# First tiles of a fused convolution and feed-forward kernel: one DMA for each load, w_in in four pieces, second convolution by GpSimd alone

## The chip, the cores and the metric

The kernel runs on one core of one Trainium2 chip. The metric is the device time of one execution in microseconds (us). Before the change it was 1414.38 us, the median of three runs (1413.4 to 1414.79 us).

## What is computed

Everything is float32. Sixteen thousand tokens (4 sequences of 4096) of width 192 go through a causal convolution whose seven taps differ for each token and each of eight heads, and then through a feed-forward layer with a rational activation:

```python
w = softmax(weight_gen)                      # over the 7 taps, per token and head
x_pad = concatenate([zeros(B, 6, D), x])     # each sequence starts with six zero tokens
out = einsum('bshk,bskhg->bshg', w, x_unf)   # x_unf: the seven tokens up to this one
h = out @ w_in                               # 192 -> 2048
P = a[0] + a[1]*h + a[2]*h**2 + a[3]*h**3
Q = 1 + |b[0]|*|h| + |b[1]|*h**2
return (P / (Q + 1e-6)) @ w_out              # 2048 -> 192
```

## The kernel before

**Layout.** Partition p of the 128 holds 128 consecutive tokens; a tile is four of them on every partition (512 tokens), and there are 32 tiles. To convolve a tile the kernel needs its four tokens and the six before them, a window of ten tokens (`xwin`, two buffers). From the third tile on, a window is one DMA of ten consecutive tokens of each partition's row (`load_x`, L273). For the first tile the six tokens before it belong to the neighbouring partition's row, or are zeros where a sequence starts. So the first tile is loaded by one DMA of four tokens (L262) and four DMAs of six tokens, each over 31 partitions (`load_halo`, L245); the second tile by one DMA of eight tokens (L267) and four of two tokens over 31 partitions. DVE writes the zeros first (L511, L512).

**First product.** x and w_in are each split into a high and a low fp32r part, and h is the sum of five products of such parts (L680). Row `wi_stage[:, 0]` holds the first 128 input rows of w_in and `wi_stage[:, 1]` the last 64 twice. It is loaded in two halves of the 2048 units, three DMAs each (`load_wi`, L254). For each half ACT copies the high part (`wi_hi`, L438), and DVE subtracts it to get the low part (`wi_lo`, L563).

**Groups.** The 16 chunks of 128 units go in six groups q of 3, 2, 3, 3, 2 and 3 chunks. For each group PE makes h in PSUM, ACT makes |h| (L474, or L479), a square (L477) and a linear term (L482), DVE finishes the numerator (L623, L626, whose end, `h_used`, frees the PSUM banks), and the denominator is summed by a DMA that GpSimd issues (groups 0, 2, 3, 5: `den` plus `beta`, L350) or by GpSimd and DVE (groups 1, 4: L357, L631). ACT inverts it two groups later (Ln L455, Exp L458), DVE forms the gate three groups later (L607), and PE multiplies it with w_out four groups later (`back`, L690).

**Convolution.** Each tile's convolution has 13 steps, seven products (L327) and six additions (L331). GpSimd does them for tile t + 2 in between its work for the groups of tile t. Only the first two tiles are convolved ahead of the loop, and there the 32 heads of a partition's four tokens are split: DVE takes 22 of the first tile (528 columns) and 12 of the second (288 columns) in `pre_conv` (L545, L556), GpSimd the rest (240 and 480 columns). The convolved tile is transposed by PE in two parts: `transpose1` (L665) and `transpose0` (L658). ACT then copies their high parts (`hi_part1` L424, `hi_part0` L419) and DVE makes the low parts (L575, L569).

**What sets the order ahead of the loop.** Each engine runs its instructions in program order, with semaphores between them.

- SP: taps 0 and 1, tokens of tile 0, its four halo DMAs, taps 2 (after `pre_sub` 1, the first taps' subtraction), first half of w_in, tokens and halos of tile 1, second half, w_out, taps 3, and the window of tile 2 once the first convolution is over. The window of tile 3 waits for the second convolution.
- DVE: softmax start (L519 maximum, L522 subtraction) for tiles 0 and 1, softmax end (L529, L532, L534) for both, `pre_conv(0)`, three tiny instructions for `root` (L585 to L590), `wi_lo` of the first half, softmax start of tile 2, the low parts of tile 0, `wi_lo` of the second half, softmax end of tile 2, `pre_conv(1)`, and then tile 0's groups.
- ACT: exponentials of taps 0 and 1 (L414), small values, both halves of `wi_hi`, high parts of tile 0, the exponential of taps 2 (which waits for `pre_sub` 3, L441), and then tile 0's groups.
- GpSimd: its part of convolutions 0 and 1, and then tile 0's groups with convolution 2.
- PE: the transposes of tile 0 after both parts of convolution 0, then the groups. In the first tile, the group with number `FIRST_XT1` = 2 begins with `transpose1` of tile 1, after both parts of convolution 1, and `hi_part1` on ACT and `lo_part1` on DVE stand one group earlier (L484, L616).

Every group q of 2 or more in tile 0 waits on PE for `h_used` of the group two before it (L705).

Of the kernel before, what the change touches and what calls it, by code (L numbers as in the profile page):

```python
# [18 lines left out]


# [6 lines left out]
ALU = mybir.AluOpType  # L27
# [18 lines left out]
FIRST_XT1 = 2  # L46


def conv_rational_ffn(nc, x, weight_gen, w_in, w_out, a, b, out):
    B, S, D = x.shape  # L50
    HEADS, TAPS = weight_gen.shape[2:]
    HEAD_DIM = D // HEADS
    FF = w_in.shape[1]
# [12 lines left out]
    SEQ_PARTS = S // PER_PART  # L66
    assert sum(GROUP_CHUNKS) == CHUNKS and D1 == 64 and COLS == 512

    x_rows = x.rearrange("b s d -> (b s d)")
    x_part = x_rows.rearrange("(p e) -> p e", p=P)  # L70
# [3 lines left out]
    def before(tokens):  # L74

        start = (PER_PART - tokens) * D
        return x_rows[start:start + (P - 1) * PER_PART * D].rearrange("(p e) -> p e", p=P - 1)[:, 0:tokens * D]

    ctx = ExitStack()
    with ctx:  # L80
# [72 lines left out]
        wi_loaded = [sem(f"wi_loaded{n}") for n in range(2)]  # L153
# [5 lines left out]
        halo_zero = sem("halo_zero")  # L159
# [47 lines left out]
        def after_dmas(s, parity, more=0):  # L207


            return 8 * s + (16 - 8 * parity + 16 * more)  # L210
# [20 lines left out]
        DVE_HEADS = (22 * NH // 32, 12 * NH // 32)  # L231
        SEQS = P // SEQ_PARTS
        HALO_DMAS = SEQS

# [4 lines left out]
        def _(sp):  # L239
            def load_halo(n, tokens):  # L240

                sp.wait_ge(halo_zero, n + 1)
                for q in range(SEQS):
                    rows = slice(q * SEQ_PARTS + 1, (q + 1) * SEQ_PARTS)
                    sp.dma_start(xwin[n][rows, 0:tokens * D],  # L245
                                 before(tokens)[rows.start - 1:rows.stop - 1, :]).then_inc(x_loaded[n], 16)

            def load_wi(half):

                units = slice(half * FF // 2, (half + 1) * FF // 2)  # L250
                for to, frm in ((wi_stage[:, 0, units], w_in[0:P, units]),
                                (wi_stage[0:D1, 1, units], w_in[P:D, units]),
                                (wi_stage[D1:P, 1, units], w_in[P:D, units])):
                    sp.dma_start(to, frm).then_inc(wi_loaded[half], 16)  # L254
# [4 lines left out]
            ahead = HALO - TOK  # L259
            sp.dma_start(taps_raw[0][:, :], taps_part[:, 0:TAPW]).then_inc(taps_loaded[0], 16)  # L260
            sp.dma_start(taps_raw[1][:, :], taps_part[:, TAPW:2 * TAPW]).then_inc(taps_loaded[1], 16)
            sp.dma_start(xwin[0][:, HALO * D:], x_part[:, 0:ROW]).then_inc(x_loaded[0], 16)  # L262
            load_halo(0, HALO)
            sp.wait_ge(pre_sub, 1)
            load_taps(2, 0)
            load_wi(0)
            sp.dma_start(xwin[1][:, ahead * D:], x_part[:, 0:2 * ROW]).then_inc(x_loaded[1], 16)  # L267
            load_halo(1, ahead)
            load_wi(1)
            sp.dma_start(wo[:, :, :], w_out.rearrange("(c p) d -> p c d", p=P)).then_inc(wo_loaded, 16)  # L270

            def load_x(s, parity):
                sp.dma_start(xwin[parity][:, :],  # L273
                             x_part[:, bass.ds(s * ROW - HALO * D, (TOK + HALO) * D)]).then_inc(x_loaded[parity], 16)

            sp.wait_ge(pre_sub, 2)
            load_taps(3, 1)
            sp.wait_ge(conv_steps, CONV_STEPS)
# [7 lines left out]
            def tile(t, odd, first=False, more_x=True, more_taps=True):  # L286
# [6 lines left out]
                if more_x:  # L293
                    sp.wait_ge(conv_steps, CONV_STEPS * (t + 2))
                    if first:
                        sp.wait_ge(conv_by_dve, 2 * CONV_STEPS)
                    load_x(t + 3, 1 - odd)
# [15 lines left out]
        def _(pool):  # L313
# [58 lines left out]
            def tile(t, odd, first=False, conv_ahead=True, taps_ahead=True):  # L372
                done = CONV_STEPS * (t + 2)
                start = 1 if first else 0
                for q in range(GROUPS):
# [8 lines left out]
                    if conv_ahead:  # L384
                        if q == start:
# [4 lines left out]
                            pool.wait_ge(x_loaded[odd], after_dmas(t + 2, odd, HALO_DMAS))  # L390
# [17 lines left out]
        def _(act):  # L408
# [26 lines left out]
            for half in range(2):  # L435
                units = slice(half * FF // 2, (half + 1) * FF // 2)
                act.wait_ge(wi_loaded[half], 3 * 16)
                act.activation(wi_hi[:, :, units], wi_stage[:, :, units], ACT.Copy).then_inc(wi_hi_ready, 1)  # L438
# [21 lines left out]
            def tile(t, odd, first=False, second=False, xt_ahead=True, taps_ahead=True):  # L460
                for q in range(GROUPS):
# [18 lines left out]
                    if first and q == 0:  # L480
                        act.wait_ge(wi_lo_ready, 2)
# [27 lines left out]
        def _(dve):  # L509

            dve.memset(xwin[0][:, 0:HALO * D], 0.0).then_inc(halo_zero, 1)  # L511
            dve.memset(xwin[1][:, 0:(HALO - TOK) * D], 0.0).then_inc(halo_zero, 1)  # L512
# [24 lines left out]
            def pre_conv(s):  # L537

                count = DVE_HEADS[s]
                cols = slice(0, count * HEAD_DIM)  # L540
                done = s * CONV_STEPS

                def product(k):
                    to = heads(dprod[k % 3]) if k else heads(conv[s])
                    dve.tensor_tensor(to[:, 0:count, :], shifted(xwin[s], k)[:, 0:count, :],  # L545
                                      tap(taps[s], k)[:, 0:count, :], ALU.mult).then_inc(conv_by_dve, 1)
# [218 lines left out]
```

## Time and profile before

| | before |
|---|---|
| median of the runs | 1414.38 us |
| the profiled execution, its own time | 1414.09 us |
| its span, first to last instruction | 1412.3 us |
| PE / ACT / DVE / GpSimd busy, share of the span | 93% / 89% / 85% / 74% |
| granted TensorE clock, mean | 0.993 of full |
| bytes moved by DMA | 152.21 MB |

The profile is of one execution; its times are counted from the span's start. Busy shares are averages over the whole span, and say nothing about how the first 100 us differ from the rest. "L245" is line 245 of the kernel. PE stands for TensorE's matmuls and transposes, PEld for its weight loads, POOL for GpSimd, SPq for the issuing of DMAs by SyncE.

### The profile page before, as it was taken

The numbers are of one execution on the slowest core, as the hardware profiler recorded it, in microseconds if no ns is written. First come the engines' busy times: TensorE is split into PE (matmuls) and PEld (weight loads), VectorE is DVE, ScalarE is ACT, GpSimd is POOL, SyncE is SP. The second block draws the span as 40 slices with busy tenths as digits, with TensorE's granted clock in tenths as the row PEclk, the third lists the DMA queues.
The fourth block names the chain that finished last, engine by engine and source line by source line (L and its number), as shares of the span: only waits on it lengthen the run. The fifth ranks groups of instructions, "written<-read, shape, count | busy, mean of one in ns | idle before, by whom it ended". The sixth has DMA issues, their size and how long they took to land.

```text
span 1412.3 us, 19121 instructions
## 1 busy us (share of the span) xinstructions
PE 1307.0 (93%) x6912; PEld 1174.9 (83%) x6912; DVE 1201.9 (85%) x841; ACT 1253.8 (89%) x1030; POOL 1040.7 (74%) x672
## 2 busy tenths in 40 slices
PE   0279999999999999999999999999999999999997
PEld 0268898888889888889888888988888898888887
DVE  2989888888988889988888998888889888899775
ACT  0379999999999999999999999999999999999995
POOL 1879787778878778877877887877788787787210
PEclk9889999999999999999999999999999999999999
DMA  2445544544545554454454455445445445533432
GB/s 89 134 93 119 115 112 109 131 93 98 131 101 117 117 126 87 109 129 97 109 131 113 88 121 114 112 109 131 93 97 131 103 115 117 123 84 78 100 68 67
DMA packets 35486, 152.21 MB, mean 108 GB/s; under 512 B 3992, under 2 KB 10260, under 8 KB 35472
## 3 DMA queue, kind: packets, MB, share of 16 engines
q0 software_dynamic: 18432, 100.67, 36.1%
q1 hardware_dynamic: 16752, 51.36, 10.9%
q8 instruction: 7, 0.11, 0.0%
q14 instruction: 7, 0.06, 0.0%
q10 hardware_dynamic: 288, 0.00, 0.0%
HBM read 38.78 MB, written 12.58 MB: 36 GB/s over the span
## 4 chain that ended last, share of the span: by engine, by line
PE 62%; ACT 26%; issue 7%; SPq 2%; DVE 2%; POOL 1%; DMA 1%; ACTq 0%; DVEq 0%; POOLq 0%
PE ops L690 32%; PE hps L680 28%; ACT num L482 7%; ACT beta L477 6%; ACT den L455 5%; ACT den L474 4%; ACT out_sb L449 2%; SPq L245 1%; PE hps L665 1%; DMA num<-in_moe_w_in 1%; SPq L254 1%; ACT den L458 1%; DVE gate L545 0%; POOL conv L331 0%; POOL prod L327 0%
## 5 line engine op out<-in xcount | busy, mean ns | idle before, releaser
L690 PE MATMUL ops<-wo,gate 128*128 128x192 f32 x4096 | 700.7, 327 | 33.0 <-ACT out_sb L449 29.4
L690 PEld LDWEIGHTS ops<-wo,gate 128*128 128x128 f32 x4096 | 674.4, 190 | 60.3 <-issue 42.0
L623 DVE TENSOR_TENSOR num<-num,hps 128x1536 f32<-128x1536 f32 (+1 forms) x192 | 301.5, 1570 | 157.6 <-ACT num L482 157.6
L331 POOL TENSOR_TENSOR conv<-conv,prod 128x768 f32<-128x768 f32 (+2 forms) x192 | 396.2, 2064 | 15.0
L607 DVE SCALAR_TENSOR_TENSOR gate<-num,coef,den 128x1536 f32<-128x1536 f32 (+1 forms) x192 | 402.8, 2098 | 2.4 <-issue 1.4
L327 POOL TENSOR_TENSOR prod<-xwin,taps 128x768 f32<-128x768 f32 (+2 forms) x192 | 334.1, 1740 | 3.5
L626 DVE SCALAR_TENSOR_TENSOR num<-num,coef,hps 128x1536 f32<-128x1536 f32 (+1 forms) x192 | 314.2, 1637 | 6.8
L350 POOL DMA_DIRECT2D den<-beta x128 | 112.9, 882 | 256.6 <-ACT beta L477 248.7
L482 ACT ACTIVATE num<-hps,coef 128x1536 f32<-128x1536 f32 (+1 forms) x192 | 288.6, 1503 | 0.0
L474 ACT ACTIVATE den<-hps,absb 128x1536 f32<-128x1536 f32 x128 | 197.1, 1540 | 87.1 <-PE hps L680 87.1
L458 ACT ACTIVATE den<-den 128x1536 f32<-128x1536 f32 (+1 forms) x192 | 259.4, 1351 | 4.2
L455 ACT ACTIVATE den<-den 128x1536 f32<-128x1536 f32 (+1 forms) x192 | 261.0, 1360 | 0.0
L680 PE MATMUL hps<-xt_hi,wi_hi 128*128 128x512 f32 x512 | 226.3, 442 | 3.9 <-ACT xt_hi L419 3.9
L680 PE MATMUL hps<-xt_hi,wi_lo 128*128 128x512 f32 x512 | 203.8, 398 | 0.0
L680 PE MATMUL hps<-xt_hl,wi_hi 128*128 128x512 f32 x512 | 203.3, 397 | 0.0
L680 PE MATMUL hps<-xt_lo,wi_hi 128*128 128x512 f32 x512 | 202.7, 396 | 0.0
L680 PE MATMUL hps<-xt_hl,wi_lo 128*128 128x512 f32 x512 | 202.2, 395 | 0.0
L477 ACT ACTIVATE beta<-hps,root 128x1536 f32<-128x1536 f32 x128 | 197.1, 1540 | 0.0
L357 POOL TENSOR_SCALAR beta<-den,absb 128x1024 f32<-128x1024 f32 x64 | 139.4, 2179 | 38.2 <-ACT den L479 22.2
L680 PEld LDWEIGHTS hps<-xt_hl,wi_hi 128*128 128x128 f32 x512 | 96.8, 189 | 24.1
L680 PEld LDWEIGHTS hps<-xt_lo,wi_hi 128*128 128x128 f32 x512 | 96.6, 189 | 24.2 <-DVE xt_lo L569 0.4
L680 PEld LDWEIGHTS hps<-xt_hl,wi_lo 128*128 128x128 f32 x512 | 96.7, 189 | 22.9
(50 smaller groups left out, 728.9 us busy)
## 6 DMA issues: line engine op xcount, KB each, us to landing
den<-beta POOLq DMA_DIRECT2D x128, 768.0 KB, 5.8
xwin<-in_x SPq DMA_DIRECT2D x30, 960.0 KB
out<-out_sb SPq DMA_DIRECT2D x32, 384.0 KB, 4.2
taps_raw<-in_weight_gen SPq DMA_DIRECT2D x32, 112.0 KB, 3.9
wo<-in_moe_w_out SPq DMA_DIRECT2D x1, 1536.0 KB, 14.9
num<-in_moe_w_in SPq DMA_DIRECT2D x2, 512.0 KB, 6.8
num<-in_moe_w_in SPq DMA_DIRECT2D x4, 256.0 KB, 8.7
xwin<-in_x SPq DMA_DIRECT2D x1, 768.0 KB
```

Source lines behind the costliest of these rows:

```text
L327: pool.tensor_tensor(to[:, first_head:, :], shifted(xwin[parity], k)[:, first_head:, :], tap(taps[parity], k)[:, first_head:, :], ALU.mult ...
L331: pool.tensor_tensor(conv[parity][:, cols], conv[parity][:, cols], prod[k % 2][:, cols], ALU.add).then_inc(conv_steps, 1)
L455: act.activation(slot(den, g), slot(den, g), ACT.Ln, bias=1.0 + 1e-6).then_inc(ln_ready, 1)
L458: act.activation(slot(den, g), slot(den, g), ACT.Exp, scale=-1.0).then_inc(inv_q_ready, 1)
L474: act.activation(slot(den, g), h_of(q), ACT.Abs, scale=absb[:, 0:1]).then_inc(abs_ready, 1)
L477: act.activation(slot(beta, g), h_of(q), ACT.Square, scale=root[:, 2:3]).then_inc(square_ready, 1)
L482: act.activation(slot(num, g), h_of(q), ACT.Identity, scale=coef[:, 3:4], bias=coef[:, 2:3]).then_inc(lin_ready, 1)
L607: dve.scalar_tensor_tensor(slot(gate, g), slot(num, g), coef[:, 0:1], slot(den, g), ALU.add, ALU.mult).then_inc(gate_ready, 1)
L623: dve.tensor_tensor(slot(num, g), slot(num, g), h_of(q), ALU.mult).then_inc(num2_ready, 1)
L626: dve.scalar_tensor_tensor(slot(num, g), slot(num, g), coef[:, 1:2], h_of(q), ALU.add, ALU.mult).then_inc(h_used, 1)
L680: last = pe.matmul(to, w, xt[:, :], start=(m == 0), stop=(m == len(terms) - 1))
L690: last = pe.matmul(ops[:, j // 2, (j % 2) * D:(j % 2 + 1) * D], gate[:, g % GATE_RING, n * COLS + j * P:n * COLS + (j + 1) * P], wo[:, c, ...
```

## The change

The host code in `kernel()` now builds two arrays before the launch: `x_windows`, in which each partition's row is its 128 tokens with the six before them (zeros at the start of a sequence) ahead of them, and `stacked(w_in)`, in which the last 64 rows stand twice, beside the first 128. All loads of x are then one DMA of ten tokens from each row, and w_in is loaded in four pieces of 512 units, one DMA each. The zeros, the halo DMAs and their waits go. The order of SP's loads, the split of the first two convolutions, DVE's order and `FIRST_XT1` change as shown.

```diff
-FIRST_XT1 = 2
+FIRST_XT1 = 3
...
+    PIECES = 4
+    PIECE = FF // PIECES
...
-        DVE_HEADS = (22 * NH // 32, 12 * NH // 32)
+        DVE_HEADS = 22 * NH // 32
...
+            def load_wi(piece):
+                units = slice(piece * PIECE, (piece + 1) * PIECE)
+                sp.dma_start(wi_stage[:, :, units], w_in[:, :, units]).then_inc(wi_loaded[piece], 16)
+
+            def load_x(s, parity):
+                sp.dma_start(xwin[parity][:, :],
+                             x_windows[:, bass.ds(s * ROW, (TOK + HALO) * D)]).then_inc(x_loaded[parity], 16)
...
+            load_taps(0, 0)
+            load_x(0, 0)
+            load_taps(1, 1)
+            load_wi(0)
+            load_wi(1)
+            load_x(1, 1)
+            load_wi(2)
+            load_wi(3)
             sp.wait_ge(pre_sub, 1)
             load_taps(2, 0)
...
             sp.wait_ge(pre_sub, 2)
             load_taps(3, 1)
+            sp.dma_start(wo[:, :, :], w_out.rearrange("(c p) d -> p c d", p=P)).then_inc(wo_loaded, 16)
             sp.wait_ge(conv_steps, CONV_STEPS)
             sp.wait_ge(conv_by_dve, CONV_STEPS)
             load_x(2, 0)
...
             for s in range(2):
                 pool.wait_ge(pre_taps, s + 1)
-                pool.wait_ge(halo_zero, 2)
-                pool.wait_ge(x_loaded[s], after_dmas(s, s, HALO_DMAS))
+                pool.wait_ge(x_loaded[s], after_dmas(s, s))
                 for n in range(CONV_STEPS):
-                    conv_step(s, n, s, s * CONV_STEPS, DVE_HEADS[s])
+                    conv_step(s, n, s, s * CONV_STEPS, DVE_HEADS if s == 0 else 0)
...
+            for piece in range(PIECES):
+                units = slice(piece * PIECE, (piece + 1) * PIECE)
+                act.wait_ge(wi_loaded[piece], 16)
                 act.activation(wi_hi[:, :, units], wi_stage[:, :, units], ACT.Copy).then_inc(wi_hi_ready, 1)
...
                     if first and q == 0:
-                        act.wait_ge(wi_lo_ready, 2)
+                        act.wait_ge(wi_lo_ready, PIECES)
...
-            dve.memset(xwin[0][:, 0:HALO * D], 0.0).then_inc(halo_zero, 1)
-            dve.memset(xwin[1][:, 0:(HALO - TOK) * D], 0.0).then_inc(halo_zero, 1)
...
             pre_softmax_end(0, 0)
             pre_softmax_end(1, 1)
-            pre_conv(0)
+            pre_conv()
+            wi_lo_piece(0)
+            lo_part1(0, 0, hps[:, BANK1, :])
+            lo_part0(0, 0)
             dve.wait_ge(root_guess, 1)
...
-            wi_lo_half(0)
+            for piece in range(1, PIECES):
+                wi_lo_piece(piece)
             dve.wait_ge(conv_steps, CONV_STEPS)
             pre_softmax_start(2, 0)
-            lo_part1(0, 0, hps[:, BANK1, :])
-            lo_part0(0, 0)
-            wi_lo_half(1)
             pre_softmax_end(2, 0)
-            pre_conv(1)
...
                 for n in range(GROUP_CHUNKS[q]):
+                    if first:
+                        pe.wait_ge(wi_lo_ready, (GROUP_START[q] + n) * P // PIECE + 1)
...
+def windows_of(x):
+    B, S, D = x.shape
+    per_part = B * S // P
+    padded = np.zeros((B, S + HALO_TOKENS, D), x.dtype)
+    padded[:, HALO_TOKENS:] = x
+    rows = [padded[n, s:s + per_part + HALO_TOKENS] for n in range(B) for s in range(0, S, per_part)]
+    return np.stack(rows).reshape(P, (per_part + HALO_TOKENS) * D)
+
+def stacked(w_in):
+    return np.stack([w_in[0:P], np.concatenate([w_in[P:], w_in[P:]])], axis=1)
```

PE's and SP's waits for DVE's part of the second convolution go too. `pre_conv()` is `pre_conv(0)` under another name.

## Rows read from the trace of the kernel before

**Rows 1.** The chain that ended last, stretches 0 to 110 and 100 to 200: start, us, what.

```profile
37.31 11.21 DMA num<-in_moe_w_in
...
69.25 1.76 DVE num L623
...
109.11 0.60 PE hps L665 x4
...
150.88 0.44 PE hps L665 x4
```

**Rows 2.** Busy time by stretch, first row: the columns' names.

```profile
core 0: us, PE busy (x) PEld busy (x) DVE busy (x) ACT busy (x) POOL busy (x), PEclk, DMA share, GB/s
...
24.00:26.00 2.00, 0.00 (x0) 0.00 (x0) 0.00 (x0) 0.00 (x0) 0.00 (x0) 1.00 0.06 25
...
120.00:162.90 42.90, 42.15 (x226) 37.79 (x225) 38.57 (x27) 40.34 (x34) 35.26 (x23) 1.00 0.48 109
```

**Rows 3.** Instructions in order of time, the start: start, us, engine, operation [idle before].

```profile
5.60 0.39 DVE L519 TENSOR_REDUCE tap_max<-taps_raw 128x32 f32<-128x224 f32 x1 [1.28 <-DMA taps_raw<-in_weight_gen]
...
8.30 0.39 DVE L534 TENSOR_TENSOR taps<-taps,tap_inv 128x224 f32<-128x224 f32 x1
```

**Rows 4.** DMA rate in 40 slices of the stretch 108 to 124.

```profile
GB/s 0 0 0 0 0 269 38 173 461 422 422 442 353 230 215 200 230 215 215 169 230 138 41 0 0 0 0 0 0 0 0 20 0 0 0 0 0 0 0 0
```

**Rows 5.** Instructions in order of time, first convolution and what follows it.

```profile
31.61 0.71 DVE L545 TENSOR_TENSOR conv<-xwin,taps 128x528 f32<-128x528 f32 x1 [22.92 <-DMA xwin<-in_x]
...
42.88 2.22 DVE L556 TENSOR_TENSOR conv<-conv,gate 128x528 f32<-128x528 f32 x2
...
44.61 1.03 POOL L331 TENSOR_TENSOR conv<-conv,prod 128x240 f32<-128x240 f32 x1
...
45.76 2.28 DVE L563 TENSOR_TENSOR wi_lo<-num,wi_hi 128x2048 fp32r<-128x2048 f32 x1
...
50.16 1.20 POOL L331 TENSOR_TENSOR conv<-conv,prod 128x480 f32<-128x480 f32 x1
...
50.97 0.69 DVE L575 TENSOR_TENSOR xt_hl<-hps,xt_hl 64x512 fp32r<-64x512 f32 x1 [1.79 <-ACT xt_hl L424]
...
52.30 2.31 DVE L563 TENSOR_TENSOR wi_lo<-num,wi_hi 128x2048 fp32r<-128x2048 f32 x1
...
52.54 3.14 POOL L331 TENSOR_TENSOR conv<-conv,prod 128x480 f32<-128x480 f32 x1
...
57.15 1.54 ACT L474 ACTIVATE den<-hps,absb 128x1536 f32<-128x1536 f32 x1 [5.46 <-PE hps L680]
```

**Rows 6.** Instructions in order of time, 65 to 100.

```profile
65.91 1.00 POOL L350 DMA_DIRECT2D den<-beta  x1
...
73.30 0.57 POOL L382 TENSOR_TENSOR taps<-taps_raw,tap_max 128x224 f32<-128x224 f32 x1 [5.14 <-DVE tap_max L634]
73.84 1.54 POOL L327 TENSOR_TENSOR conv<-xwin,taps 128x768 f32<-128x768 f32 x1
...
77.08 1.85 POOL L331 TENSOR_TENSOR conv<-conv,prod 128x768 f32<-128x768 f32 x1
...
78.51 1.55 ACT L474 ACTIVATE den<-hps,absb 128x1536 f32<-128x1536 f32 x1 [3.85 <-PE hps L680]
...
82.09 0.89 POOL L350 DMA_DIRECT2D den<-beta  x1 [3.16 <-ACT beta L477]
...
82.89 1.49 ACT L455 ACTIVATE den<-den 128x1536 f32<-128x1536 f32 x1
...
85.92 1.54 ACT L474 ACTIVATE den<-hps,absb 128x1536 f32<-128x1536 f32 x1
...
89.48 0.88 POOL L350 DMA_DIRECT2D den<-beta  x1 [3.02 <-ACT beta L477]
```

**Rows 7.** GpSimd's DMA at 110.97, from issue to landing.

```profile
DMA to landing us min/median/max: 8.0/8.0/8.0
```

More of the change, by code:

```diff
@@ L21 @@
+import numpy as np
 import concourse.bass as bass
@@ L45, with conv_rational_ffn @@
 XT0, XT1 = 4, 1
-FIRST_XT1 = 2
-def conv_rational_ffn(nc, x, weight_gen, w_in, w_out, a, b, out):
-    B, S, D = x.shape
+FIRST_XT1 = 3
+def conv_rational_ffn(nc, x_windows, weight_gen, w_in, w_out, a, b, out):
+    B, S = weight_gen.shape[:2]
+    D = w_out.shape[1]
     HEADS, TAPS = weight_gen.shape[2:]
     HEAD_DIM = D // HEADS
-    FF = w_in.shape[1]
+    FF = w_in.shape[2]
     PER_PART = B * S // P
@@ L152, in conv_rational_ffn @@
         small_loaded = sem("small_loaded")
-        wi_loaded = [sem(f"wi_loaded{n}") for n in range(2)]
+        wi_loaded = [sem(f"wi_loaded{n}") for n in range(PIECES)]
         wo_loaded = sem("wo_loaded")
@@ L205, in conv_rational_ffn, with after_dmas @@
         pe_passed = sem("pe_passed")
-        def after_dmas(s, parity, more=0):
-            return 8 * s + (16 - 8 * parity + 16 * more)
+        def after_dmas(s, parity):
+            return 8 * s + (16 - 8 * parity)
         def wait_q(engine, t, q):
@@ L239, in _ @@
         def _(sp):
[L240 to L254, printed above, removed]
+            def load_wi(piece):
+                units = slice(piece * PIECE, (piece + 1) * PIECE)
+                sp.dma_start(wi_stage[:, :, units], w_in[:, :, units]).then_inc(wi_loaded[piece], 16)
@@ L268, in _ @@
[L268 to L274, printed above, removed]
             sp.wait_ge(pre_sub, 2)
             load_taps(3, 1)
+            sp.dma_start(wo[:, :, :], w_out.rearrange("(c p) d -> p c d", p=P)).then_inc(wo_loaded, 16)
@@ L554, in pre_conv, with wi_lo_piece @@
                         product(k + 1)
-                    dve.wait_ge(conv_by_dve, done + 2 * k)
-                    dve.tensor_tensor(conv[s][:, cols], conv[s][:, cols], dprod[k % 3][:, cols],
+                    dve.wait_ge(conv_by_dve, 2 * k)
+                    dve.tensor_tensor(conv[0][:, cols], conv[0][:, cols], dprod[k % 3][:, cols],
                                       ALU.add).then_inc(conv_by_dve, 1)
-            def wi_lo_half(half):
-                units = slice(half * FF // 2, (half + 1) * FF // 2)
-                dve.wait_ge(wi_hi_ready, half + 1)
+            def wi_lo_piece(piece):
+                units = slice(piece * PIECE, (piece + 1) * PIECE)
+                dve.wait_ge(wi_hi_ready, piece + 1)
                 dve.tensor_tensor(wi_lo[:, :, units], wi_stage[:, :, units], wi_hi[:, :, units].bitcast(F32),
@@ L677, in first_product @@
                     for m, (w, xt) in enumerate(terms):
-                        if very_first and n == 0 and m == 2:
+                        if first and q == 0 and n == 0 and m == 2:
                             pe.wait_ge(xt_lo_ready, 2)
@@ L705, in tile @@
                         pe.wait_ge(h_used, i - 1)
-                    if first and GROUP_START[q] == CHUNKS // 2:
-                        pe.wait_ge(wi_lo_ready, 2)
                     if xt_ahead and q == (FIRST_XT1 if first else XT1):
                         pe.wait_ge(conv_steps, CONV_STEPS * (t + 2))
-                        if first:
-                            pe.wait_ge(conv_by_dve, 2 * CONV_STEPS)
                         pe.sem_inc(pe_passed, 1)
@@ L717, in tile @@
                         transpose0(1 - odd)
-                    first_product(q, odd, first and q == 0)
+                    first_product(q, odd, first)
                     if first and q == LAG:
@@ L754 @@
     nc = bacc.Bacc("TRN2", target_bir_lowering=False, num_devices=1)
+    B, S, D = inputs["x"].shape
+    laid_out = {"x_windows": windows_of(inputs["x"]), "weight_gen": inputs["weight_gen"],
+                "w_in": stacked(inputs["moe_w_in"]), "w_out": inputs["moe_w_out"],
+                "a": inputs["moe_a"], "b": inputs["moe_b"]}
     arrays, args = {}, []
-    for name in _INS:
-        v = np.ascontiguousarray(inputs[name])
+    for name, value in laid_out.items():
+        v = np.ascontiguousarray(value)
         arrays[f"in_{name}"] = v
         args.append(nc.dram_tensor(f"in_{name}", v.shape, mybir.dt.from_np(v.dtype), kind="ExternalInput").ap())
-    B, S, D = inputs["x"].shape
     out = nc.dram_tensor("out_0", (B * S, D), F32, kind="ExternalOutput").ap()
```

46 lines of the change are left out of this document (10 added, 36 removed).

## The prediction, made before the changed kernel was run

> **What bounds the kernel now.** Two parts have to be told apart. In the body, PE is the bound: between 120 and 163 us it is busy for 42.15 of 42.90 us at full clock [rows 2], and the chain of waits goes through the transposes of a new tile at 109.11 and again at 150.88 [rows 1], so a tile costs 41.8 us there. The diff leaves a tile's instructions in the body alone: the loads of x keep their size, and only their source rows move. So I look at the part ahead of it, and read the chain, then the stretches, then the instructions in order of time.
>
> The start is bound by loads. Both engines start the first convolution at about 31.6 us, and DVE had been idle for 22.92 us, until x came [rows 5]. Between 24 and 26 us no engine works, and the DMA engines move 25 GB/s at a share of 0.06, one sixteenth [rows 2]: the halo DMAs of 31 partitions run on one of 16 engines. Behind them SP can't issue, so w_in is late too: its last DMA lands 11.21 us after 37.31, at 48.5 us, and the chain passes through it [rows 1]. After that comes DVE's share of the second convolution, which holds its first work on group 0 of tile 0 until 69.25 us [rows 1], though ACT had begun that group at 57.15 [rows 5]. ACT gets group 2 at 78.51 [rows 6], and from there the same sequence runs into the body. So every us by which ACT reaches group 3 (85.92 [rows 6]) earlier should come off the span, as long as GpSimd keeps up.
>
> **The change, part by part.** All times below are from the span's start.
>
> Loads. Taps 0, x of tile 0 (960 KB) and taps 1 are issued first, each on 128 partitions. Before, taps 1 had landed at 5.60 with a 384 KB load of x beside it [rows 3]. Now 0.59 MB more lies ahead of it; a window of this size, just after SP issued it, moved at 422 GB/s and more [rows 4], which makes 1.4 us, and it is issued one place later, some 0.4 us. I take 7.3 us; bounds are 5.6 us (as before) and 9.6 us (the extra bytes at half that rate, and everything late by another 1.1 us). The Trainium skill (DMA: Bandwidth & Descriptors, Anatomy of one DMA) fits a GpSimd DMA as 2.0 us plus bytes at 436 GB/s; as an estimate, the 1.2 MB up to taps 1 would be there at 5.5 us, and the sum would gain 1.8 us more. The first rows of this trace speak against taking it, since 112 KB took until 5.60.
>
> The rest of the loads (w_in in 2 MB, the second window, some 3 MB in all) needs 7 us at 422 GB/s and 15 at half of that. All of it is there by 23 us at the latest, before anything below asks for it; its cover is the first convolution. w_out comes later still, but is asked for only at group 4. The two zeroings on DVE (1.4 us) were hidden behind the taps, so taking them away is worth nothing.
>
> First convolution. From taps 1 at 5.60 to the end of the second softmax at 8.69 are 3.1 us [rows 3]: DVE starts at 10.4 instead of 31.61. GpSimd needs only the first softmax and starts some 1.1 us sooner. The two engines hold each other up: a DVE step takes 0.71 us with GpSimd idle and 1.1 beside it, and a GpSimd addition of 480 columns took 3.14 us instead of 1.20 when it met the 2.31 us of `wi_lo` [rows 5]. So they take turns. DVE's 13 steps took from 31.61 to 45.10, 13.5 us [rows 5]. GpSimd, two steps ahead, finishes at 10.4 + 14.0 - 2.0 = 22.4 and goes on to full width, so DVE's last two steps wait for steps of 1.6 us instead of 0.5: 1.0 us more. DVE ends at 24.9.
>
> DVE's queue after it. It is now on the path, since ACT's first work on tile 0 stands behind the exponential of taps 2, which waits for DVE's subtraction of taps 2, which stands behind all four pieces of `wi_lo`. A piece takes half of 2.28 us [rows 5], 1.15, and each waits for a full-width step of GpSimd (product 1.62 from start to start, addition 1.93 [rows 6]). Piece 0: 1.25 + 1.15, to 27.3. Low parts of tile 0: 1.33, from 50.97 to 52.30 [rows 5], to 28.6; PE and ACT have made the transposes and high parts meanwhile. `root`: 0.66, from 45.10 to 45.76 [rows 5], to 29.3. Pieces 1 to 3: three turns of 1.15 + 1.7, less some of the first wait, 8.2, to 37.5. Maximum, wait and subtraction: 1.9, to 39.4. Exponential 0.4: ACT starts group 0 at 39.9 instead of 57.15.
>
> Tile 0. Group 0 takes ACT 4.4 us (78.51 to 82.89 for three such operations [rows 6]), so DVE starts its numerator at 44.3; its convolution no longer stands in the way (before: 69.25). From there to ACT's group 2 were 9.26 us, with 0.60 for the transposes of tile 1 [rows 1, 6], which now come a group later: 8.7, so 53.0 against 78.51. From group 2 to group 3 were 7.41 us (78.51 to 85.92 [rows 6]); now ACT's high part of tile 1 (0.6) stands between: group 3 starts at 61.0 against 85.92. **That is 24.9 us earlier.**
>
> GpSimd. Its second convolution is 7 products and 6 additions of full width: 7 x 1.62 + 6 x 1.93 = 22.9 us. Four pieces of `wi_lo` add 0.9 each (1.94 us were added by one of twice the size [rows 5]) and DVE's last two steps 0.35 each: 27.3, from 22.4 to 49.7. Its DMA for group 0 stands behind that. Such DMAs land after 5.8 us usually, but after 8.0 when a window of x was issued just before [rows 7], and here SP issues tile 3's window at the same moment: 57.7. ACT wants it after group 2, at 53.0 + 4.4 + 0.6 = 58.0. So it is just in time, and this is what is late next. After it, GpSimd starts the third convolution at 52.5 (of the 7.4 us from its DMA at 65.91 to 73.30, 5.14 were a wait [rows 6]), which is 3.6 us late against 73.84 - 24.9; its next waits for ACT, 3.16 and 3.02 us [rows 6], take that up.
>
> Sum: 1414.09 (the profiled execution's own time) - 24.9 = 1389.2 us. That execution lay 0.3 us under the median, so no correction.
>
> **The rivals.**
>
> *No holding up.* If DVE doesn't wait for GpSimd's full-width steps, DVE's queue loses 1.0 + 1.25 + 4.7 + 1.5 = 8.4 us. GpSimd then ends at 22.4 + 22.9 = 45.3, its DMA lands at 53.3 and becomes the bound: 4.7 us more gained, 1384.5; with a landing after 6.5 us, 1383.0. The rows of the first convolution and of 3.14 us speak against it; for it speaks only that the turns might fall better than I drew them.
>
> *GpSimd decides.* If each of the 13 steps is held as the ones beside `wi_lo` are, the convolution takes 22.9 + 13 x 0.9 = 34.6 us and ends at 57.0, the DMA lands at 65.0, and ACT waits 7 us for it: 1396.2. DVE has little to do between 40 and 44 us, which speaks against so much.
>
> *The new load goes to one DMA engine,* as the halos do: then 983 KB at 25 GB/s [rows 2] take 39 us, x of tile 0 is there at 42.5 instead of 31.6, everything shifts by 32 us against my sum, and the kernel ends at 1421.3, slower. It decides from a landing of about 35 us on. Against it: the same shape in the body moved at 422 GB/s [rows 4]. The Trainium skill (DMA: Bandwidth & Descriptors, Why a DMA increments its semaphore by 16 and not by 1) says that a DMA goes to the largest number of engines up to 16 which divides its outer dimension, 1 for 31 rows and 16 for 128; the share of 0.06 agrees, and by it this rival doesn't happen.
>
> *The start is hidden anyway.* If the body had idle time to absorb it, nothing would change: 1414. PE at 98% leaves no room [rows 2].
>
> **How the numbers follow.** Forecast 0.55, no holding up 0.20, GpSimd decides 0.20, one engine 0.03, hidden 0.02. The range runs from 1383.5 to 1396.5 and holds the bounds of the landing (-1.7 and +2.3 us) within the first three cases. A measurement here tells 0.2% (2.8 us) from no change; the first three cases are all beyond that: faster 0.95, same 0.02, slower 0.03.
>
> **What would show it.** In the profile after: DVE's first convolution step near 10 us; no stretch of 25 GB/s; `wi_lo` steps longer than 1.15 us, with GpSimd steps between; ACT's first `den` of tile 0 near 40 us, its idle time before the exponential of taps 2 ended by DVE's subtraction; the last step of GpSimd's second convolution near 50 us; ACT's `den` of group 3 near 61; tile periods unchanged at 41.8 us. It is wrong if the first `den` comes near 31 (no holding up), if ACT's first Ln waits long for GpSimd's DMA (GpSimd decides), or if a later tile loses what the start gained.

## The result, and the profile after

The changed kernel takes 1391.74 us (median of four runs, 1391.33 to 1392.87), against 1414.17 us for the kernel before: a ratio of 0.9843, 95% interval 0.9826 to 0.986. That is 22.4 us less; 24.9 were forecast, and 1391.74 lies in the range of 1383.5 to 1396.5. The profiled execution had a span of 1391.0 us and took 1392.87 us itself, the slowest of the four; the last section says why. Two executions further below, one of kernel E and one of the kernel before beside it, took over 1900 us at a granted clock of 0.66 and are left out of the medians.

The first rows to read are the changed kernel's first 24 us (busy time by stretch; the columns are those of [rows 2]).

```profile
2.00:4.00 2.00, 0.00 (x0) 0.00 (x0) 0.00 (x0) 0.03 (x1) 0.00 (x0) 1.00 0.73 106
4.00:6.00 2.00, 0.00 (x0) 0.00 (x0) 0.78 (x2) 0.39 (x1) 0.00 (x0) 1.00 0.85 327
6.00:8.00 2.00, 0.00 (x0) 0.00 (x0) 0.00 (x0) 0.00 (x0) 0.00 (x0) 1.00 0.96 314
...
10.00:12.00 2.00, 0.00 (x0) 0.00 (x0) 1.90 (x6) 0.86 (x3) 1.32 (x2) 1.00 1.02 397
...
20.00:22.00 2.00, 0.00 (x0) 0.00 (x0) 2.00 (x3) 0.00 (x0) 1.84 (x3) 1.00 0.56 181
22.00:24.00 2.00, 0.00 (x0) 0.00 (x0) 2.00 (x3) 0.00 (x0) 1.92 (x3) 1.00 0.02 7
```

The stretches of 25 GB/s at a share of 0.06 are gone: the DMA engines are nearly full until almost everything has come, at about 22 us. SP isn't held up behind the halos any more either. In the kernel before, the issue of one load of taps behind them had taken 5.38 us, where the first loads took 0.4 us each:

```profile
8.55 5.38 SPq L257 DMA_DIRECT2D taps_raw<-in_weight_gen  x1
```

The instructions in order of time show what the engines made of it.

```profile
8.56 0.39 DVE L494 TENSOR_REDUCE tap_max<-taps_raw 128x32 f32<-128x224 f32 x1 [3.74 <-DMA taps_raw<-in_weight_gen]
...
11.57 1.11 DVE L518 TENSOR_TENSOR conv<-xwin,taps 128x528 f32<-128x528 f32 x1
...
23.34 3.15 DVE L529 TENSOR_TENSOR conv<-conv,gate 128x528 f32<-128x528 f32 x2
23.93 2.00 POOL L305 TENSOR_TENSOR conv<-xwin,taps 128x768 f32<-128x768 f32 x1
...
26.42 2.56 DVE L536 TENSOR_TENSOR wi_lo<-num,wi_hi 128x1024 fp32r<-128x1024 f32 x1
...
30.85 7.77 DVE L536 TENSOR_TENSOR wi_lo<-num,wi_hi 128x1024 fp32r<-128x1024 f32 x3
...
40.85 1.52 ACT L451 ACTIVATE den<-hps,absb 128x1536 f32<-128x1536 f32 x1
...
45.43 1.75 DVE L595 TENSOR_TENSOR num<-num,hps 128x1536 f32<-128x1536 f32 x1 [3.15 <-ACT num L459]
...
49.16 1.83 POOL L309 TENSOR_TENSOR conv<-conv,prod 128x768 f32<-128x768 f32 x1
...
50.92 1.01 POOL L327 DMA_DIRECT2D den<-beta  x1
```

DVE's first step of the convolution stood at 31.61 before [rows 5] and is at 11.57 now. The last two steps of its share take 3.15 us for the two, where they took 2.22 beside GpSimd's short steps. A piece of `wi_lo` takes 2.56 us and three take 7.77, for 1.15 us of work each: DVE and GpSimd lengthen each other, as if they took turns. The chain that ended last says what decides after that (start, us, what).

```profile
49.92 1.01 issue
50.92 9.70 DMA den<-beta
60.62 0.02 issue
60.64 1.48 ACT den L432
...
63.78 1.43 ACT den L451
...
71.80 1.19 POOL beta L334
72.99 2.49 POOL prod L305
...
84.90 1.82 POOL conv L309
86.73 0.14 issue
86.86 0.60 PE hps L637 x4
```

It runs through GpSimd's second convolution, then 9.70 us of the DMA of group 0, then ACT, and from 71.80 through GpSimd again to the transposes of tile 2 at 86.86, which came at 109.11 before [rows 1]: 22.25 us earlier. From there on both kernels do the same in the same time, 41.5 us from one copy of an output tile to the next, up to the last tile. That one takes 32.3 us in this trace and 31.0 in that of before, so that about 1 us of the gain is missing again at the end of this execution.

### The profile page after: what moved, and what is told of

It is laid out like the page before. It is cut to its first block, busy times and chain, and to the rows that moved or that the text cites. A ratio compares the mean times of both kernels' runs of the same rounds, so it can differ in the third digit from the quotient of the medians.

```text
span 1391.0 us, 19098 instructions
## 1 busy us (share of the span) xinstructions
PE 1310.3 (94%) x6912; PEld 1177.7 (85%) x6912; DVE 1194.8 (86%) x828; ACT 1253.9 (90%) x1032; POOL 1046.6 (75%) x672
## 4 chain that ended last, share of the span: by engine, by line
PE 62%; ACT 26%; issue 7%; POOL 4%; DMA 1%; DVE 0%; SPq 0%; ACTq 0%; POOLq 0%; DVEq 0%
PE ops L664 33%; PE hps L654 28%; ACT num L459 7%; ACT beta L454 6%; ACT den L432 6%; ACT den L451 4%; POOL conv L309 2%; ACT out_sb L426 2%; POOL prod L305 2%; PE hps L637 1%; DMA den<-beta 1%; ACT den L435 1%; DMA taps_raw<-in_weight_gen 0%; ACT taps L391 0%; POOL conv L305 0%
## 5 line engine op out<-in xcount | busy, mean ns | idle before, releaser
L664 PE MATMUL ops<-wo,gate 128*128 128x192 f32 x4096 | 702.1, 328 | 32.8 <-ACT out_sb L426 29.3
L595 DVE TENSOR_TENSOR num<-num,hps 128x1536 f32<-128x1536 f32 (+1 forms) x192 | 301.5, 1570 | 158.8 <-ACT num L459 158.7
L309 POOL TENSOR_TENSOR conv<-conv,prod 128x768 f32<-128x768 f32 (+1 forms) x192 | 399.7, 2082 | 15.0
L579 DVE SCALAR_TENSOR_TENSOR gate<-num,coef,den 128x1536 f32<-128x1536 f32 (+1 forms) x192 | 402.4, 2096 | 2.7 <-issue 1.3
L305 POOL TENSOR_TENSOR prod<-xwin,taps 128x768 f32<-128x768 f32 (+1 forms) x192 | 338.7, 1764 | 3.4
L654 PEld LDWEIGHTS hps<-xt_hi,wi_hi 128*128 128x128 f32 x512 | 97.5, 190 | 27.1 <-DVE num L598 11.4
```

What stands on the lines that cost most here:

```text
L305: pool.tensor_tensor(to[:, first_head:, :], shifted(xwin[parity], k)[:, first_head:, :], tap(taps[parity], k)[:, first_head:, :], ALU.mult ...
L309: pool.tensor_tensor(conv[parity][:, cols], conv[parity][:, cols], prod[k % 2][:, cols], ALU.add).then_inc(conv_steps, 1)
L579: dve.scalar_tensor_tensor(slot(gate, g), slot(num, g), coef[:, 0:1], slot(den, g), ALU.add, ALU.mult).then_inc(gate_ready, 1)
L595: dve.tensor_tensor(slot(num, g), slot(num, g), h_of(q), ALU.mult).then_inc(num2_ready, 1)
L654: last = pe.matmul(to, w, xt[:, :], start=(m == 0), stop=(m == len(terms) - 1))
L664: last = pe.matmul(ops[:, j // 2, (j % 2) * D:(j % 2 + 1) * D], gate[:, g % GATE_RING, n * COLS + j * P:n * COLS + (j + 1) * P], wo[:, c, ...
```

## Experiments

Ten more kernels were run, each beside the kernel before, and the changed kernel and K a second time (mostly five executions each; eleven of P, four of EF). The medians are blurred by the last tile, so the traces are read at two marks: the transposes of tile 2 ("T2"), and ACT's first copy of an output tile ("copy"), which closes the start. A group's `den` is the start of ACT's first instruction on it. All times in us:

| kernel | median | first conv. step | group 0's den | group 2's den | group 0's DMA: issue, landing after | group 3's den | T2 | copy |
|---|---|---|---|---|---|---|---|---|
| before | 1414.17 | 31.61 | 57.15 | 78.51 | 65.91, 6.5 | 85.92 | 109.11 | 132.28 |
| changed | 1391.74 | 11.57 | 40.85 | 54.22 | 50.92, 9.7 | 63.69 | 86.86 | 110.04 |
| changed, again | 1392.08 | 11.70 | 40.97 | 55.80 | 51.05, 10.0 | 64.09 | 87.45 | 110.60 |
| A loads alone | 1391.74 | 9.47 | 36.22 | 57.39 | 43.17, 6.1 | 64.80 | 88.10 | 111.25 |
| P GpSimd alone | 1414.45 | 31.87 | 58.19 | 79.42 | 72.71, 9.9 | 86.82 | 110.03 | 133.21 |
| B split back | 1392.95 | 11.58 | 38.10 | 57.98 | 43.76, 5.9 | 65.86 | 90.50 | 113.67 |
| C taps 1 first | 1390.35 | 9.41 | 37.77 | 52.23 | 49.63, 9.7 | 62.43 | 85.57 | 108.72 |
| D tile 3's x later | 1389.42 | 11.61 | 40.88 | 55.67 | 50.96, 5.9 | 63.55 | 87.26 | 110.39 |
| E softmax early | 1392.77 | 11.41 | 35.47 | 52.13 | 50.66, 9.8 | 63.49 | 86.63 | 109.79 |
| F DMA early | 1391.94 | 11.51 | 40.78 | 55.39 | 44.38, 5.9 | 63.27 | 86.90 | 110.08 |
| EF both | 1393.45 | 11.51 | 35.97 | 51.10 | 43.74, 5.9 | 58.98 | 86.85 | 111.43 |
| I beta on ACT | 1392.02 | 11.49 | 40.75 | 55.44 | 50.83, 10.0 | 63.86 | 87.04 | 110.20 |
| K all four | 1391.93 | 9.72 | 33.29 | 50.84 | 40.70, 5.9 | 58.72 | 82.19 | 105.35 |
| K again | 1390.60 | 9.43 | 32.75 | 48.12 | 40.75, 5.9 | 57.30 | 84.54 | 110.38 |

Two yardsticks for small differences. The kernel before had a median of 1413.67 us beside A to D, 1414.72 beside P, E, F and EF, 1414.00 beside I and K, and 1414.51 beside the two repeats, so medians of different rounds differ by up to 1 us for no reason of the kernel. And the two traces of the changed kernel differ by 0.6 us at T2 and at the copy, and by 1.6 us at group 2's `den`; what is smaller than that in one trace is not a finding.

**A. The loads alone,** in the kernel before.

```diff
-            load_halo(0, HALO)
+            load_taps(0, 0)
+            load_taps(1, 1)
+            load_x(0, 0)
             sp.wait_ge(pre_sub, 1)
             load_taps(2, 0)
             load_wi(0)
...
+            load_x(1, 1)
             load_wi(1)
```

`x_windows` and `stacked(w_in)` are built as in the changed kernel, but w_in comes in two halves, one DMA each.

> The kernel before with its loads changed alone: windows and stacked w_in, one DMA each, in the old order (taps 0, taps 1, x of tile 0, taps 2, w_in in two halves around x of tile 1). The split of the second convolution, DVE's order and FIRST_XT1 = 2 stay. My theory (two chains: DVE's queue ahead of tile 0, and GpSimd's second convolution with its DMA for group 0): taps 1 lands at 5.6 us, the first convolution starts at 8.8 us instead of 31.6, the 1.8 us that ACT waited for the second half of w_in go too, and the rest of the old sequence follows unchanged, so DVE's first numerator starts at 44.5 instead of 69.25 and the kernel takes about 1389.7 us, 2 us less than with the whole change: the rest of the change costs what it gains or more. Rival (the parts are needed together, since DVE's 13 steps of the second convolution stand on the path): DVE's numerator not before 50 us, 1396 us or more.

Its median is 1391.74 us (ratio 0.984, 0.9827 to 0.9853), the very figure of the whole change. The rival falls: the numerator starts at 46.90, not after 50. The forecast was 2 us too low: taps 1 was there only at 6.4 us and x of tile 0 at 9.3, and DVE's steps of 288 columns took 1.3 to 1.5 us beside GpSimd's, where they took 0.45 alone. So the new loads carry all but about 1 us of the gain: A's T2 and copy come 0.7 to 1.2 us after those of the changed kernel's two traces. That the median is the same to the digit is chance. The rest of the diff isn't idle, though. A loads taps 1 ahead of x of tile 0, the changed kernel behind it; C below, the changed kernel with A's order of these two, has T2 and the copy 2.5 us before A. No run separates the windows of x from the stacked w_in, nor w_in's four pieces and `FIRST_XT1` = 3 from the rest.

**P. The second convolution by GpSimd alone,** in the kernel before.

```diff
-        DVE_HEADS = (22 * NH // 32, 12 * NH // 32)
+        DVE_HEADS = (22 * NH // 32, 0)
...
-            pre_conv(1)
```

PE's and SP's waits for DVE's part of it go too.

> The kernel before with one part of the change alone: the second convolution by GpSimd alone, DVE's 13 steps of it gone; loads, orders and FIRST_XT1 = 2 as before. My theory: DVE could start tile 0's numerator at 61.7 us instead of 69.25, but GpSimd's convolution, 46.4 us + 22.9 us of full-width steps + 3.4 us behind the two wi_lo, ends near 72.7 us, and the transposes of tile 1 wait for it there as they waited for the numerator before (72.97): no change, 1414 us within 1 us. Rival (DVE's queue was the bound): up to 7 us less, 1407 us.

As expected: 1414.45 against 1414.72 us, ratio 0.9998 (0.9989 to 1.0007). DVE's numerator starts at 62.79, but GpSimd ends at 72.7, and its DMA behind it, and PE's transposes, wait for that:

```profile
70.96 1.80 POOL L331 TENSOR_TENSOR conv<-conv,prod 128x768 f32<-128x768 f32 x1
72.71 1.00 POOL L350 DMA_DIRECT2D den<-beta  x1
72.83 0.61 PEld L664 LDWEIGHTS ops<-ident,conv 128*64 128x64 f32 x4 [12.79 <-issue]
```

**B. The second convolution split again,** in the changed kernel.

```diff
-                    conv_step(s, n, s, s * CONV_STEPS, DVE_HEADS if s == 0 else 0)
+                    conv_step(s, n, s, s * CONV_STEPS, DVE_HEADS[s])
...
             pre_softmax_end(2, 0)
+            pre_conv(1)
```

> The changed kernel with the second convolution split again, DVE taking 12 of 32 heads (288 columns) right after the second softmax part of tile 2, before tile 0's groups. My theory: DVE's first numerator starts some 3.5 us later (49 instead of 45.43), since DVE then works alone at about 0.45 us a step; GpSimd's part ends near 44 instead of 51, its DMA for group 0 lands in time, and ACT's wait of 1.5 us for it goes: 1393.7 us, 2 us more than the changed kernel. Rival (GpSimd's convolution alone sets the start): 1390 us or less.

1392.95 us. The steps came as expected (numerator at 48.95, DMA issued at 43.76 and landed after 5.9, no wait for it), and in its trace the copy is 3.6 us later than in the changed kernel; the median is 1.2 us above it, in the expected direction but smaller. GpSimd's convolution alone doesn't set the start. So the second convolution by GpSimd alone, worth nothing in the kernel before (P), is worth 3.1 to 3.6 us at the copy here, where DVE's 13 steps would stand ahead of its work on tile 0 and GpSimd's longer convolution is nearly hidden.

**C. Taps 1 before x.** Two lines of SP's list change places.

```diff
-            load_x(0, 0)
             load_taps(1, 1)
+            load_x(0, 0)
```

> The changed kernel with taps 1 issued before x of tile 0. My theory: taps 1 lands at 5.6 us instead of 8.5, x of tile 0 at about 8.6; both engines start the first convolution near 8.7 us; DVE starts 2.8 us earlier, GpSimd 1.9 us earlier and without its lead of one step, so DVE's last steps no longer meet full-width steps. The chain through GpSimd is 1.7 to 2.5 us shorter: 1389.7 us. Rival (x of tile 0 lands only at 10 us or later, and the taps were not what the start waited for): 1391.5 us.

Taps 1 is there at 6.1 instead of 8.6, x of tile 0 at 9.4, and the whole start moves by 1.3 us (T2 at 85.57, copy at 108.72); the median is 1390.35. Expected were 1.7 to 2.5; x comes later than I took it to, and now the convolution waits for it.

**D. Tile 3's window later.**

```diff
                     sp.wait_ge(conv_steps, CONV_STEPS * (t + 2))
+                    if first:
+                        sp.wait_ge(q_by_dma[0], 16)
                     load_x(t + 3, 1 - odd)
```

> The changed kernel, but SP issues the window of tile 3 only after the DMA of group 0 has landed, so that the two don't collide. My theory: that DMA lands after 6 us instead of 9.7, ACT's first Ln no longer waits for it (1.5 us), and then DVE's queue is the bound: 1.5 us less, 1390.2 us. Rival (GpSimd's chain alone decides, ACT follows it at once): 3.7 us less, 1388.0 us. Second rival (the collision is with something else, as w_out's or the taps' loads): DMA still over 8 us, no change.

The collision is what made the landing late: 5.9 us instead of 9.7, with the window and the taps behind it both issued after it, and ACT's first Ln doesn't wait any more. But group 2's `den`, which the landing can't touch, came 1.45 us later than in the changed kernel's first trace, so T2 and the copy are no earlier. Busy time by stretch shows why. The changed kernel:

```profile
50.00:52.00 2.00, 2.00 (x6) 1.52 (x6) 1.74 (x2) 0.00 (x0) 2.00 (x3) 0.50 0.15 15
52.00:54.00 2.00, 2.00 (x10) 1.55 (x9) 0.78 (x1) 0.00 (x0) 2.00 (x3) 0.99 0.86 184
```

and D:

```profile
50.00:52.00 2.00, 2.00 (x6) 1.52 (x6) 1.77 (x2) 0.00 (x0) 2.00 (x3) 0.50 0.00 0
52.00:54.00 2.00, 2.00 (x7) 1.52 (x6) 0.76 (x1) 0.00 (x0) 2.00 (x3) 0.50 0.85 169
```

In the second stretch the granted clock is 0.99 in one and 0.50 in the other, and 10 matmuls fall into it or 7. PE had been idle for 11 us before, and its 15 matmuls of group 2 begin at 1.2 GHz in both; when 2.4 GHz comes back differs from run to run. It isn't D's doing: in the changed kernel's own second trace the 15 matmuls took 6.5 us, as in D, where they had taken 5.1 in the first, and ACT waited only 0.28 us for the DMA instead of 1.46. Against that trace D reaches group 3 0.5 us earlier and T2 and the copy 0.2. The median, 1389.42, is 2.3 us below the changed kernel's; three of D's five executions (1388.8 to 1389.4) lie below all nine of the changed kernel (lowest 1390.8), the other two at 1392.6 and 1392.9, and the trace is of the last. The trace settles the collision, and the run times don't settle the gain.

**E, F and EF. Each chain shortened alone, and both.** E moves DVE's softmax start of tile 2 ahead of `wi_lo` pieces 1 to 3. F lets GpSimd issue the DMA of group 0 (`group(0, 0, 0, True)`) inside its second convolution, whose loop stands behind the definition of `group` there. EF is both. E's lines stand first below, F's behind them.

```diff
+            dve.wait_ge(conv_steps, CONV_STEPS)
+            pre_softmax_start(2, 0)
             for piece in range(1, PIECES):
                 wi_lo_piece(piece)
-            dve.wait_ge(conv_steps, CONV_STEPS)
-            pre_softmax_start(2, 0)
...
                     conv_step(s, n, s, s * CONV_STEPS, DVE_HEADS if s == 0 else 0)
+                    if s == 1 and n == 8:
+                        group(0, 0, 0, True)
...
-                    group(t, odd, q, first)
+                    if not first or q > 0:
+                        group(t, odd, q, first)
```

> The changed kernel with DVE's softmax start of tile 2 ahead of wi_lo pieces 1 to 3 instead of behind them. ACT's first den of tile 0 then comes at about 36 us instead of 40.85, but its linear term still waits for the fourth piece, so DVE's first numerator starts some 2 us earlier, at 43. My theory: ACT's first Ln waits for GpSimd's DMA of group 0, which lands at 60.6 as before, so nothing is gained: 1391.7 us within 0.5. Rival (DVE's queue ahead of tile 0 is the bound): 2.2 us less, 1389.5 us.

> The changed kernel with GpSimd issuing the DMA of group 0 after the ninth of the 13 steps of its second convolution instead of after all. My theory: it is issued near 44 us, lands near 50, ACT's first Ln doesn't wait (1.5 us less), the convolution ends 0.7 us later at no cost, and DVE's queue is then the bound: 1390.2 us, as with the window of tile 3 issued later. Rival (GpSimd's chain alone decides): 3 us or more less.

> The changed kernel with both: softmax start of tile 2 ahead of wi_lo pieces 1 to 3, and the DMA of group 0 after the ninth step. My theory of two chains nearly level: the first alone gives nothing, the second alone 1.5 us, both together 1.5 + 2.2 = 3.7 us, 1388.0 us. Rival (a third limit, GpSimd's later work or the TensorE clock, follows at once): together no more than the second alone, 1390.2 us.

E: ACT starts group 0 at 35.47 and then waits 3.36 us for the DMA, where it had waited 1.46; T2 stays (86.63), and the median is no lower (1392.77). The queue of DVE alone is not the bound. F: no wait for the DMA, but group 2 came 1.2 us later (its 15 products took 6.3 us instead of 5.1, at half clock for longer, as in D), so 0.4 us at group 3, nothing at T2 (86.90), and 1391.94; I had expected 1.5 less. The changed kernel's second trace has group 2 later still, so here too the clock hides what the edit is worth. EF: together they bring group 3 to 58.98, 4.7 us earlier, and still T2 stands at 86.85, and the median is 1393.45. My theory of two chains falls, and its rival, a third limit, holds. The waits and the instructions of EF name it:

```profile
65.19 0.86 POOL L320 DMA_DIRECT2D den<-beta  x1
65.80 1.83 POOL L305 TENSOR_TENSOR prod<-xwin,taps 128x768 f32<-128x768 f32 x1
67.70 2.90 POOL L309 TENSOR_TENSOR conv<-conv,prod 128x768 f32<-128x768 f32 x1
...
76.14 2.94 POOL L305 TENSOR_TENSOR prod<-xwin,taps 128x768 f32<-128x768 f32 x1
...
81.86 2.95 POOL L305 TENSOR_TENSOR prod<-xwin,taps 128x768 f32<-128x768 f32 x1
```

GpSimd has no wait left: it used to stand 3.3 us before the DMA of group 3 (67.22 in the changed kernel) and now comes there at 65.19 without standing. From that DMA to T2 it needs 19.6 us in the kernel before, the changed one, C and E, and 21.7 in EF, since its steps met more of DVE's instructions (2.9 us for steps that take 1.5 to 1.9 alone). That ACT's and DVE's lead is what put them there is argued, not shown: K's first trace, with as much lead, needed 19.9 us. PE, early too, waits for GpSimd and loses its clock:

```profile
86.85 1.03 PE L640 MATMUL hps<-ident,conv 128*64 128x128 f32 x4 [3.42 <-POOL conv L309]
```

```profile
84.00:86.00 2.00, 0.00 (x0) 0.00 (x0) 0.67 (x1) 2.00 (x2) 1.92 (x2) 1.00 0.01 0
86.00:88.00 2.00, 1.15 (x5) 1.07 (x6) 1.96 (x2) 1.39 (x3) 2.00 (x4) 0.64 0.26 23
88.00:90.00 2.00, 2.00 (x6) 1.52 (x6) 1.94 (x4) 0.51 (x1) 1.92 (x3) 0.51 0.79 215
```

After the idle time the granted clock is half until 90, where the changed kernel, which reached the same transposes 0.38 us ahead of GpSimd, kept 1.00; the transposes take 1.03 us instead of 0.60, and the copy comes 1.4 us later than in the changed kernel's first trace (0.8 than in its second).

**I and K. GpSimd's work shortened.** I gives the beta of group 1 in tile 0 to ACT. K is I with C, E and F (the DMA after the eighth step instead of the ninth).

```diff
-                    group(t, odd, q, first)
+                    if not first or q != 1:
+                        group(t, odd, q, first)
...
                         act.activation(slot(den, g), h_of(q), ACT.Abs).then_inc(abs_ready, 1)
+                        if first and q == 1:
+                            act.wait_ge(abs_ready, 2)
+                            act.activation(slot(beta, g), slot(den, g), ACT.Identity, scale=absb[:, 1:2],
+                                           bias=absb[:, 0:1]).then_inc(beta_by_pool, 1)
```

> The changed kernel with 1.2 us of work taken off GpSimd in tile 0: ACT computes beta of group 1 while it has nothing else. My theory after the first eight runs (two chains that meet when GpSimd issues the DMA of group 3, where GpSimd waits 3.3 us for ACT, and ACT's chain hangs on the landing of group 0's DMA at 60.6): the 1.2 us only lengthen that wait; ACT's first copy of an output tile, which closes the start, comes at 110.0 as before, 1391.7 us within 0.7. Rival (GpSimd's work from the first convolution to the transposes of tile 2 is one unbroken chain): 1.2 us less, 108.8.

> Four edits to the changed kernel together: taps 1 loaded first, softmax start of tile 2 ahead of wi_lo pieces 1 to 3, the DMA of group 0 after the eighth step of the second convolution, beta of group 1 on ACT. With the first two edits for ACT's chain in place, GpSimd has no wait left and its work is the bound until the transposes of tile 2 (86.85 with the second and third edit alone): less 1.3 for the earlier start and 1.2 for beta, they come at 84.3, and ACT's first copy of an output tile at 107.5, 2.5 us before the changed kernel's: 1389.2 us. Rival (PE, waiting for those transposes, falls to half clock again, as with the second and third edit, where this cost 1.4 us): first copy at 108.9, 1390.6 us.

I: as expected, 1392.02 us, copy at 110.20, and GpSimd's wait before the DMA of group 3 grew from 3.3 to 4.0 us. K's first trace has T2 at 82.19 and the copy at 105.35, 2.1 us before what I had expected and 4.7 us before the changed kernel's, and that execution took 1387.38 us. Yet the median of its five is 1391.93, not 1389.2. The changed kernel and K were run once more:

> The changed kernel once more, unaltered, beside the next kernel on one chip. My theory: its start repeats (ACT's first copy of an output tile within 1.5 us of 110.0), and its runs spread over 3 us because the last tile takes between 29.3 and 32.3 us, by whether the TensorE clock is full or half there: 1391.7 us within 1. Rival (the start itself varies by 3 us): first copy 2 us or more away from 110.0.

> The kernel with all four edits once more, for a second trace and five more runs beside the changed kernel. My theory: its first copy of an output tile comes near 105.4 again, 4.7 us before the changed kernel's, and its median, blurred by the last tile's clock, is 3 to 4.7 us below the changed kernel's on this chip. Rival (its transposes of tile 2 sometimes find TensorE idle and at half clock, as with two of the edits alone): first copy at 107 or later, and a median within 1.5 us of the changed kernel's.

The changed kernel repeats (110.60, 1392.08). K doesn't. The turns of DVE and GpSimd fell otherwise, so that DVE's first numerator started at 39.32 instead of 41.12, and PE's 15 matmuls of group 2 took 5.1 us instead of 6.0; ACT was at group 2 at 48.12 instead of 50.84. GpSimd then met more of DVE's instructions (2.94 and 2.95 again), and T2 found PE idle for 4.93 us and at half clock. The chain of the second trace shows it:

```profile
79.55 2.95 POOL prod L305
...
82.58 1.82 POOL conv L309
84.40 0.14 issue
84.54 1.03 PE hps L644 x4
85.57 4.26 PE hps L661 x10
```

Ten products take 4.26 us where they took 2.33, and the copy is at 110.38, no better than the changed kernel's. Over ten runs K's median is 1390.7, over nine the changed kernel's is 1391.9: a difference of 1.2 us that the spread (1387.4 to 1393.6, and 1390.8 to 1393.4) doesn't carry. No version tried beats the changed kernel reliably; C is the simplest with a gain in its trace.

## Why the prediction was right

**Loads.** Right in kind: the loads were the bound, and the new ones use all DMA engines. Taps 1 landed at 8.5 us, not 7.3, within the bounds of 5.6 to 9.6; the whole start is 1.2 us later for it. The sum counted only the bytes ahead of taps 1, at 422 GB/s. The rows above show 327 and 314 GB/s, and some 1.5 MB moved by 8 us, more than the 1.2 MB up to taps 1: the pieces of w_in issued behind it had a share already.

**First convolution and turns.** Right: DVE started 1.2 us later than drawn and ended 1.6 later (its first step took 1.11 us instead of 0.71, since GpSimd was at work already), with 0.9 of the 1.0 us foreseen for its last two steps. The rival without holding up is out: by it, ACT's first `den` would have come near 31 us, and it came at 40.85 (forecast 39.9), with pieces of `wi_lo` of 2.6 us.

**Tile 0.** Group 0's numerator at 45.43 (forecast 44.3), group 2 at 54.22 (53.0): the 1.2 us of the taps carried along. Here the agreement is partly luck. The sum has no term for PE's clock after its 11 us of idle time, and in the second trace, with the numerator at 45.56, group 2 came at 55.80.

**GpSimd.** Its second convolution took 27.0 us from 23.93 to 50.9, forecast 27.3. The term that was mis-sized is the landing of its DMA: 9.7 us, not 8.0, so that ACT waited 1.46 us for it, where the sum had it just in time. That made group 3 come at 63.69 instead of 61.0: 1.2 us from the taps' landing and 1.5 from the DMA's, 2.7 in all, against the 2.5 us between 24.9 forecast and 22.4 measured. In the second trace ACT waited only 0.28 us, group 2's slower matmuls took the place of the wait, and group 3 came at 64.09.

**Slack.** The step that every us by which ACT reaches group 3 earlier should come off the span, as long as GpSimd keeps up, was right for this change only because GpSimd kept up with 3.3 us to spare. EF shows the limit: 4.7 us on ACT gave nothing. The forecast said that GpSimd is late next; it placed this at the DMA of group 0, and the runs placed a second such point at the transposes of tile 2. The tile period is unchanged, as forecast, but it is 41.5 us in both kernels, not 41.8.

**The rival in which the new load goes to one DMA engine** fell by the first 22 us of the trace. **"GpSimd decides"** didn't happen: the convolution took 27.0 us, not 34.6. Its sign, ACT's first Ln waiting for the DMA, did appear, at 1.46 us instead of 7, and came from the landing.

## What to carry to other kernels

Read a slow start by the DMA share before the engines: a share of 0.06 means one engine of sixteen, and a load over 31 partitions ran there at 25 GB/s, with the loads behind it held as well; laying out the sources so that each load is one DMA over 128 partitions was worth 21 to 22 us. When three engines' chains are level within 3 us, shortening one or two can give nothing, as E, F and EF did: change one at a time and read a mark at the end of the stretch, not at the edited place. And an engine made early can make the next one lose: TensorE, arriving before its data, waited (3.4 us in EF, 4.9 in K's second trace) and went on at half clock.

## What the runs showed of the hardware

**The last tile takes 29.3 to 32.3 us by TensorE's clock.** PE has little to do from 1370 on, while ACT and DVE finish the last groups, and in some executions the granted clock then falls to half (1.2 GHz) for the last products. Busy time by stretch at the end, the changed kernel:

```profile
1370.00:1375.00 5.00, 1.49 (x6) 1.29 (x5) 4.82 (x4) 4.94 (x5) 0.00 (x0) 0.80 0.50 98
1375.00:1380.00 5.00, 5.00 (x18) 5.00 (x17) 1.82 (x1) 1.10 (x1) 0.00 (x0) 0.52 0.00 0
```

and kernel F:

```profile
1370.00:1375.00 5.00, 1.49 (x9) 1.20 (x8) 4.91 (x4) 4.94 (x5) 0.00 (x0) 1.00 0.50 98
1375.00:1380.00 5.00, 5.00 (x33) 5.00 (x32) 1.82 (x1) 1.19 (x1) 0.00 (x0) 1.00 0.01 3
```

The same 5 us hold 18 matmuls in one and 33 in the other, after the same 1.49 us of work in the 5 us ahead. F's profiled execution took 1389.98 us, the changed kernel's 1392.87, with the copy at 110.08 and 110.04. The changed kernel's own two traces differ in the same way: the last tile took 32.3 us in one and 29.3 in the other, and the executions 1392.87 and 1390.84 us, with the copy at 110.04 and 110.60. From the first copy to the last but one all fourteen traces take 1245.1 to 1245.6 us, so the start and the last tile make up every difference between them. For the executions without a trace this is argued from their mean clock only (0.991 to 0.993 for the changed kernel). Medians of five can hardly tell apart versions that differ by less than the last tile does.

**An accumulating DMA of 768 KB** from GpSimd, that of group 0, landed after 5.9 us where no load was issued within 5 us of it (B, D, F, EF, K), after 6.1 and 6.5 with a window of 960 KB issued 3.9 and 3.5 us behind it (A, before), and after 9.7 to 10.0 with the window issued 0.1 us behind it and a load of 112 KB 2 to 3 us later (changed, P, C, E, I).

**DVE and GpSimd lengthen each other, as if they took turns by whole instructions,** when DVE reads two operands from SBUF: a piece of `wi_lo`, 1.15 us of work, took 2.56 us, steps of 288 columns took 1.3 to 1.5 us instead of 0.45 (A, B), and GpSimd's steps of 1.5 to 1.9 us became 2.4 to 2.9. DVE's instructions with one operand in PSUM weren't lengthened: in the changed kernel's first 110 us the first part of a numerator of 1536 columns (L595) took 1.74 or 1.75 us each time beside GpSimd's work, while the gate of the same width (L579), all in SBUF, took 1.8 to 3.4.
